# Turning input and output blocks in 32x32 squares on VectorE and DMA instead of with TensorE transposes

## The chip, the cores and the metric

The kernel runs on one core of a Trainium2 chip. The metric is the time of one execution on the device in microseconds; the median of three runs is compared.

## What is computed

`x` is 2 x 4096 x 192 (float32), 8192 rows of 192 features. Three stages follow each other:

```python
# attention: 8 heads of 24 features, 7 causal taps each
w = softmax(weight_gen, axis=-1)                  # (2, 4096, 8, 7)
out = einsum('bshk,bskhg->bshg', w, windows(x))   # sum of 7 shifted, weighted rows
# layer 1: 192 -> 1536 -> 192
h = (silu(out @ w_gate) * (out @ w_val)) @ w_out
# layer 2: 192 -> 2048 -> 192
z = h @ w_in
return (z * clip(z + 3, 0, 6) / 6) @ w_out2
```

## The kernel before

**Tiling.** Partition `p` holds the 64 consecutive rows `64p` to `64p + 63`. A block is `STEPS = 4` of these per partition, 512 rows; there are `BLOCKS = 16`. The taps' sum is made on VectorE with rows on the partitions (128 x 768, 4 rows of 192 features each). The matmuls want features on the partitions and the 512 rows as columns: a main tile of features 0 to 127 and a tail tile of features 128 to 191, which is kept in both halves of the partitions. So each block's input is turned once, and its output once in the other direction, since the result comes with features on the partitions (PSUM pair `acc[2]`) and is stored by rows.

**Numbers.** Each matmul operand is split in a rounded part (`hi`, made on ScalarE by a cast) and the rest (`lo`, made on VectorE by a subtraction), and three products are added. Matmuls use half of the array's rows (64 x 128), LOW and HIGH, two at a time. A hidden tile is 128 features of the 1536 (`N1 = 12` gated tiles, two up matmul sets and a product each) or of the 2048 (`N2 = 16` plain tiles).

**Periods.** Period `i` (1 to 15) runs the 12 gated tiles of block `i` and then the 16 plain tiles of block `i - 1`, in 8 steps of two tiles (`period`, L1295). Period 0 has gated tiles alone, period 16 plain tiles alone (`last_period`, L1322). Periods 2 to 14 are a loop on the engines (L293), the others are written out. The down matmuls run `LAG = 4` tiles behind the up matmuls, woven into the same steps (`gated_step` L1002, `plain_step` L1124); a step may begin when the hidden tiles of the step before the last are made (`up_ready`, L906).

**Order on the engines.** All orders are written out by hand. For tile `n` ScalarE makes silu or relu out of PSUM (`bend`, L448; it waits for the rest of tile `n - 2`, since `hidden` has two buffers), then the cast of tile `n - 1` (`round_hi`, L459). VectorE makes the product of tile `n` (`tile_product`, L715), then slot 0, then the rest of tile `n - 1` (`tile_lo`, L727), then slot 1 (`between`, L774). The slots hold the other work:

- the 18 operations of the next block's taps (`conv_op`, L664; the last two write `conv_main` and `conv_tail`, L709 and L711), in order from tile 0 on;
- in (6, 0) the fold of the output's tail (`fold_output`, L765), which moves the others back by one;
- in (10, 0) and (10, 1) the rest of layer 2's input (`input2_lo`, L754);
- in (11, 1), (12, 0) and (12, 1) the rest of layer 1's next input out of PSUM (`input1_lo`, L739): one operation of 512 columns and four of 256 on half the partitions;
- in (17, 1) the sum of layer 1's tail (`sum_tail`, L760).

ScalarE adds after tile 4 the copies of the output (`take_sum2`, L494, with `out_main`), after tile 9 the copies of the turned output out of PSUM (`take_rows`, L502), after tile 11 the casts of the next input (`input1_hi`, `input1_tail_hi`, L469 to L486), after tile 16 the copies of layer 1's sum (`take_sum1`, L488).

**TensorE's turning.** `transpose_output(i - 2)` (L1214) follows gated tile `ROWS_AFTER = 7`, `transpose_input(i + 1)` (L1179) follows the last gated tile; each is 8 transposes of the main part and 4 of the tail, half an array each, into PSUM. Block 0 is different: its seven products are added up and turned at once by matmuls with the identity (`turn_products0`, L1237). The last block's output is turned by `transpose_last` (L1197).

**SyncE.** In the loop it waits for the rows of block `i - 2`, stores them in one DMA (`store`, L358), waits for the taps of block `i + 1` and for the store, and loads the window of block `i + 2` (L380 to L385). GpSimd only makes the weights' rests in periods 0 and 1.

Of the kernel before, what the change touches and what calls it, by code (L numbers as in the profile page):

```python
# [35 lines left out]
P = 128  # L36
# [3 lines left out]
LAG = 4  # L40
FOLD_AT = 6
ROWS_AFTER = 7
# [4 lines left out]
def swiglu_hardswish_kernel(nc, x, taps_in, w_gate, w_val, w1_out, w2_in, w2_out, out):  # L47
# [69 lines left out]
    with ExitStack() as ctx:  # L117
# [26 lines left out]
        conv_main = sb("conv_main", [P, STEPS, P])  # L144
        conv_tail = sb("conv_tail", [P, STEPS, TAIL])
# [22 lines left out]
        ident = sb("ident", [P, P])  # L168
        last_tail = mid_tail
# [14 lines left out]
        s_window = sem("s_window")  # L184
        s_stage = [sem(f"s_stage{s}") for s in range(BUFFERS)]
# [15 lines left out]
        s_out_main = sem("s_out_main")  # L201
        s_out_rows = sem("s_out_rows")
        s_last_tail = sem("s_last_tail")
# [11 lines left out]
        s_conv_rows = sem("s_conv_rows")  # L215
# [4 lines left out]
        s_out_fold = sem("s_out_fold")  # L220
        s_mid = sem("s_mid")

        s_in_cols = sem("s_in_cols")
# [5 lines left out]
        s_out_t = sem("s_out_t")  # L229
# [12 lines left out]
        def by_half(ap):  # L242
            return ap.rearrange("p (t h q) -> p t h q", h=2, q=TAIL)

        def by_parity_half(ap):
            return ap.rearrange("p (a b h q) -> p a b h q", b=2, h=2, q=TAIL)

        def main_cols(banks):
            return banks[:, :, 0:STEPS * TAIL].rearrange("p h (t q) -> p t h q", q=TAIL)

        def tail_cols(banks, rows):
            return banks[rows, :, STEPS * TAIL:D * 2].rearrange("p h (a q) -> p a h q", q=TAIL)
# [3 lines left out]
        def input_banks(b):  # L256


            return acc_pair[1 if isinstance(b, int) and b == 0 else 2]

        def tails0():

            return acc_pair[2][halves[0], :, 0:STEPS * TAIL].rearrange("p h (t q) -> p t h q", q=TAIL)

        def output_banks(b):

            return acc_pair[1 if isinstance(b, int) and b >= BLOCKS - 2 else 2]
# [42 lines left out]
        def _(sp):  # L310
# [63 lines left out]
            sp.wait_ge(s_conv_rows, 1)  # L374
# [3 lines left out]
            sp.wait_ge(s_conv_rows, 2)  # L378
# [7 lines left out]
            for b in range(BLOCKS - 4, BLOCKS - 1):  # L386
                sp.wait_ge(s_out_rows, b + 1)
                store(b)
            sp.wait_ge(s_out_rows, BLOCKS)
            sp.wait_ge(s_last_rows, 2)  # L390
            store(BLOCKS - 1)
            sp.wait_ge(s_stored, 16 * BLOCKS)
# [34 lines left out]
        def _(act):  # L427
# [46 lines left out]
            def input1_tail_hi0():  # L474
                for half in halves:
                    last = nc.scalar.copy(by_half(inp[1]["tail_hi"][half, :]), tails0())
                last.then_inc(s_in1_hi, 1)

            def input1_tail_hi(b, par):
# [889 lines left out]
```

## Time and profile before

| | |
|---|---|
| median of 3 runs | 1233.72 us (1233.35 to 1233.98) |
| the profiled execution | 1232.71 us, its span 1230.9 us |
| TensorE busy | 1212.3 us (98%) |
| VectorE busy | 870.6 us (71%) |
| ScalarE busy | 662.6 us (54%) |
| GpSimd busy | 41.1 us (3%) |
| DMA packets | 12051, 32.01 MB |
| chain that ended last | TensorE 91%, VectorE 6%, ScalarE 2%, issue 1% |
| granted TensorE clock | 1.00 |

The profile follows one execution. Busy times are sums over the whole span; a matmul's own duration (0.39 us) is longer than the distance to the next, as they are pipelined and run two at a time. In a timeline the first number is the start in us, the second the time the instruction or merged group took, a number in brackets the idle time of its engine just before it and what ended that. The chain is followed back from the last instruction.

### The profile page before, as it was taken

To read this page: it belongs to the slowest core of one execution; us is meant where nothing else is said; L and a number is where in the kernel's file an instruction comes from. 1 tells how busy PE (TensorE), PEld (TensorE's weight loads), DVE (VectorE), ACT (ScalarE), POOL (GpSimd) and SP (SyncE) were. 2 spreads that over 40 slices of the span, in tenths; PEclk is the share of its full clock that TensorE was granted. 3 is DMA by queue.
4 is the path that set the end of the run, shared out by engine and by line. 5 is a ranking of instruction groups with operands and counts; after the bars stand their busy time and mean duration, and the time that the engine had idled before them with its cause. 6 is when DMAs were issued, how large, how long until landed. Compare 5 with 4: busy or idle time off the path is not lost.

```text
span 1230.9 us, 26836 instructions
## 1 busy us (share of the span) xinstructions
PE 1212.3 (98%) x10868; PEld 1025.1 (83%) x10868; DVE 870.6 (71%) x1349; ACT 662.6 (54%) x1185; POOL 41.1 (3%) x38
## 2 busy tenths in 40 slices
PE   8989999999999999999999999999999999999998
PEld 7767688889888888888889888898888888898976
DVE  4978786776868668686776868668686776864555
ACT  4455646556454554646556454554646556454555
POOL 4431000000000000000000000000000000000000
PEclk9999999999999999999999999999999999999999
DMA  6231001010100101001010100101001010000000
GB/s 179 97 101 33 1 8 39 2 46 1 46 2 1 46 1 46 1 9 39 1 46 1 46 1 1 46 1 46 1 8 38 1 46 1 14 1 2 14 12 16
DMA packets 12051, 32.01 MB, mean 26 GB/s; under 512 B 1078, under 2 KB 5942, under 8 KB 11828
## 3 DMA queue, kind: packets, MB, share of 16 engines
q1 hardware_dynamic: 11812, 30.42, 7.5%
q8 instruction: 86, 1.41, 0.5%
q10 hardware_dynamic: 144, 0.11, 0.0%
q14 instruction: 9, 0.07, 0.0%
HBM read 24.24 MB, written 6.29 MB: 25 GB/s over the span
## 4 chain that ended last, share of the span: by engine, by line
PE 91%; DVE 6%; ACT 2%; issue 1%; POOL 0%; ACTq 0%; POOLq 0%
PE up_bank L868 34%; PE acc L883 22%; PE up_bank L874 16%; PE acc L890 15%; DVE hid_lo L729 2%; PE up_bank L1234 1%; DVE hidden L724 1%; DVE prod_even L612 1%; DVE sum_even L616 1%; DVE hidden L721 1%; ACT hidden L456 1%; PE acc L1245 0%; PE acc L1251 0%; DVE sum_odd L616 0%; DVE prod_odd L612 0%
## 5 line engine op out<-in xcount | busy, mean ns | idle before, releaser
L868 PE MATMUL up_bank<-in_hi,up_hi 64*128 64x512 f32 x1280 | 355.3, 400 | 11.1 <-DVE hidden L721 6.4
L868 PE MATMUL up_bank<-in_lo,up_hi 64*128 64x512 f32 x1280 | 346.8, 387 | 0.0
L868 PE MATMUL up_bank<-in_hi,up_lo 64*128 64x512 f32 x1280 | 346.8, 387 | 0.0
L883 PE MATMUL acc<-hid_hi,dn_hi 64*128 64x512 f32 x872 | 337.5, 387 | 0.1
L890 PE MATMUL acc<-hid_hi,dn_tail 64*128 64x512 f32 x872 | 337.5, 387 | 0.1
L883 PE MATMUL acc<-hid_lo,dn_hi 64*128 64x512 f32 x872 | 337.1, 387 | 0.0
L890 PE MATMUL acc<-hid_lo,dn_tail 64*128 64x512 f32 x872 | 336.8, 386 | 0.0
L883 PE MATMUL acc<-hid_hi,dn_lo 64*128 64x512 f32 x872 | 336.8, 386 | 0.0
L724 DVE SCALAR_TENSOR_TENSOR hidden<-hidden,up_bank 128x512 f32<-128x512 f32 x256 | 175.8, 687 | 195.9 <-ACT hidden L456 195.5
L729 DVE TENSOR_TENSOR hid_lo<-hidden,hid_hi 128x512 fp32r<-128x512 f32 x448 | 312.7, 698 | 1.5 <-ACT hid_hi L463 0.5
L456 ACT ACTIVATE hidden<-up_bank,half_col 128x512 f32<-128x512 f32 x256 | 176.1, 688 | 227.9 <-DVE hid_lo L729 214.1
L454 ACT ACTIVATE hidden<-up_bank 128x512 f32<-128x512 f32 x192 | 115.0, 599 | 298.9 <-PE up_bank L874 245.4
L463 ACT CAST hid_hi<-hidden 128x512 fp32r<-128x512 f32 x448 | 273.7, 611 | 1.5 <-DVE hidden L724 0.8
L868 PEld LDWEIGHTS up_bank<-in_hi,up_hi 64*128 64x128 f32 x1280 | 195.8, 184 | 48.7 <-DVE hidden L721 18.4
L721 DVE TENSOR_TENSOR hidden<-hidden,up_bank 128x512 f32<-128x512 f32 x192 | 131.9, 687 | 123.2 <-ACT hidden L454 113.6
L868 PEld LDWEIGHTS up_bank<-in_lo,up_hi 64*128 64x128 f32 x1280 | 196.4, 184 | 21.8 <-DVE in_lo L743 0.4
L868 PEld LDWEIGHTS up_bank<-in_hi,up_lo 64*128 64x128 f32 x1280 | 196.7, 184 | 18.0
L874 PE MATMUL up_bank<-in_tail_hi,up_tail_hi 64*128 64x512 f32 x640 | 198.0, 387 | 0.0
L874 PE MATMUL up_bank<-in_tail_hi,up_tail_lo 64*128 64x512 f32 x640 | 197.9, 386 | 0.0
L874 PE MATMUL up_bank<-in_tail_lo,up_tail_hi 64*128 64x512 f32 x640 | 197.8, 386 | 0.0
L890 PEld LDWEIGHTS acc<-hid_hi,dn_tail 64*128 64x128 f32 x872 | 160.4, 184 | 14.5 <-PE acc L883 1.0
L883 PEld LDWEIGHTS acc<-hid_hi,dn_hi 64*128 64x128 f32 x872 | 160.5, 184 | 13.9 <-DVE hid_lo L729 0.5
(130 smaller groups left out, 1459.0 us busy)
## 6 DMA issues: line engine op xcount, KB each, us to landing
window<-in_x_dram SPq DMA_DIRECT2D x14, 960.0 KB
out_dram<-out_rows SPq DMA_DIRECT2D x16, 384.0 KB, 2.4
stage<-in_moe_w_out_dram SPq DMA_DIRECT2D x7, 384.0 KB, 3.5
taps<-in_weight_gen_dram SPq DMA_DIRECT2D x1, 1456.0 KB, 8.1
stage<-in_moe_w_in_dram SPq DMA_DIRECT2D x4, 256.0 KB, 4.2
window<-in_x_dram SPq DMA_DIRECT2D x2, 472.5 KB
window<-in_x_dram SPq DMA_DIRECT2D x2, 283.5 KB
stage<-in_moe_w_gate_dram SPq DMA_DIRECT2D x2, 256.0 KB, 6.4
```

The costliest lines, as they stand in the source:

```text
L454: nc.scalar.activation(buf, up_bank[2 * (n % 2)][:, :], ACT.Silu).then_inc(s_bent, 1)
L456: nc.scalar.activation(buf, up_bank[n % 4][:, :], ACT.Relu, bias=half_col[:, 0:1], scale=1.0 / 6.0).then_inc(s_bent, 1)
L463: nc.scalar.copy(hid_hi[:, n % RING, :], hidden[:, n % 2, :]).then_inc(s_hid_hi, 1)
L612: return nc.vector.tensor_tensor(by_head(dst[:, :]), by_head(window[:, j * D:(j + STEPS) * D]), w[:, :, j:j + 1].to_broadcast([P, HEADS, G ...
L616: return nc.vector.tensor_tensor(dst[:, :], dst[:, :], src[:, :], ALU.add)
L721: nc.vector.tensor_tensor(buf, buf, up_bank[2 * (n % 2) + 1][:, :], ALU.mult).then_inc(s_hidden, 1)
L724: nc.vector.scalar_tensor_tensor(out=buf, in0=buf, scalar=1.0, in1=up_bank[n % 4][:, :], op0=ALU.min, op1=ALU.mult).then_inc(s_hidden, 1)
L729: nc.vector.tensor_tensor(hid_lo[:, n % RING, :], hidden[:, n % 2, :], as_f32(hid_hi[:, n % RING, :]), ALU.subtract).then_inc(s_hid_lo, 1)
L868: return nc.tensor.matmul(dst[:, :], w[lane[half], col:col + P], a[lane[half], :], start=first and product == 0, stop=False)
L874: return nc.tensor.matmul(dst[:, :], w[lane[half], col:col + P], a[lane[half], :], start=False, stop=product == 2)
L883: return nc.tensor.matmul(acc[y][0], w[lane[half], k, :], a[lane[half], n % RING, :], start=half == LOW and product == 0 and k == 0, stop= ...
L890: return nc.tensor.matmul(acc[y][1], dn_tail[y][lane[half], k, :], a[lane[half], n % RING, :], start=half == HIGH and product == 0 and k == 0,
```

## The change

From block 2 on the input and, up to block 14, the output are turned without TensorE. VectorE's transpose turns every 32x32 square of a tile in place; the squares are then brought to their places by DMA.

- **Input.** Operation 17 of the taps writes the whole sum into `sum_even` in one add. VectorE turns it into `in_turned` (768 columns) in slot (11, 0). SyncE writes it to a scratch in DRAM with 4 DMAs (32 partitions, 6 runs of 512 bytes each), waits for them, and reads it back with 3 (`in_main`, which shares its memory with `out_main`, and `in_tail` in both halves). ScalarE casts the two whole tiles after tiles 21 and 22, VectorE makes the rests in slots (22, 1) and (23, 1).
- **Output.** VectorE turns `acc[2][0]` out of PSUM (512 columns) in slot (6, 1), and the folded tail (256 columns) in slot (7, 0). SyncE stores the squares with 24 DMAs a block, each 32 partitions with 4 runs of 128 bytes. The copies into `out_main` and out of the turned PSUM banks go.
- **Order.** The slots (6, 0), (6, 1), (7, 0) are kept for the output in every period, the taps' operations take the others. The two exponentials of the remaining taps in period 1 move from tiles 22 and 24 to 23 and 25. The window is loaded when the last product of the taps has read the old one. SyncE's loop is written out.
- **Blocks 0, 1 and 15.** TensorE turns on in blocks 0 and 1 (block 1 now with 8 + 8 transposes) and for the last output. Columns stand in another order (by square, then step), so some copies there have other access patterns.

```diff
-ROWS_AFTER = 7
+SQ = 32
...
-        conv_main = sb("conv_main", [P, STEPS, P])
-        conv_tail = sb("conv_tail", [P, STEPS, TAIL])
+        in_turned = sb("in_turned", [P, STEPS * D])
...
+        in_tail = sb("in_tail", [P, COLS])
+        in_main = out_main
+        turned_dram = nc.dram_tensor("turned_dram", (D, COLS), F32, kind="Internal").ap()
...
+        CONV_OPS = 17
+        LAST_PRODUCT = 15
+        BROUGHT = 3 * 16
+        STORES = (P // SQ) * (D // SQ) * 16
...
+            def bring_input(b):
+
+                by_feature = turned_dram.rearrange("(e f) (j c) -> f e j c", f=SQ, c=P)
+                for j in range(P // SQ):
+                    sp.dma_start(by_feature[:, :, j, :],
+                                 in_turned[j * SQ:(j + 1) * SQ, :].rearrange("f (e c) -> f e c", c=P)
+                                 ).then_inc(s_in_dram, 16)
+                sp.wait_ge(s_in_dram, (b - 1) * (P // SQ) * 16)
+                sp.dma_start(in_main[:, :], turned_dram[0:P, :]).then_inc(s_in_cols, 16)
+                for half in halves:
+                    sp.dma_start(in_tail[half, :], turned_dram[P:D, :]).then_inc(s_in_cols, 16)
+
             def store(b):
-                sp.dma_start(out_by_p[:, bass.ds(b * (STEPS * D), STEPS * D)], out_rows[:, :]).then_inc(s_stored, 16)
+
+                rows = out_by_p[:, bass.ds(b * (STEPS * D), STEPS * D)].rearrange("(j q) (t d) -> j q t d", q=SQ, t=STEPS)
+                for j in range(P // SQ):
+                    for e in range(D // SQ):
+                        if e < P // SQ:
+                            p0, at = e * SQ, j * P
+                        else:
+                            p0, at = j % 2 * TAIL + e * SQ - P, COLS + j // 2 * P
+                        sp.dma_start(rows[j, :, :, e * SQ:(e + 1) * SQ],
+                                     out_rows[p0:p0 + SQ, at:at + P].rearrange("q (t d) -> q t d", t=STEPS)
+                                     ).then_inc(s_stored, 16)
...
-            with sp.Fori(2, BLOCKS - 2) as i:
-                sp.wait_ge(s_out_rows, i - 1)
+            sp.wait_ge(s_in_turned, 1)
+            bring_input(2)
+            for i in range(2, BLOCKS - 2):
+                sp.wait_ge(s_out_turned, 2 * i - 2)
                 store(i - 2)
-                sp.wait_ge(s_conv_rows, i + 1)
-                sp.wait_ge(s_stored, 16 * i - 16)
+                sp.wait_ge(s_conv, i * CONV_OPS + LAST_PRODUCT)
+                sp.wait_ge(s_stored, i * STORES - STORES)
                 load_window(i + 2)
+                sp.wait_ge(s_in_turned, i)
+                sp.wait_ge(s_in1_lo, 2 * i + 2)
+                bring_input(i + 1)
...
             def input1_hi(b):
-                banks = input_banks(b)
-                act.wait_ge(s_in_cols, b + 1)
-                nc.scalar.copy(by_half(inp[1]["hi"][:, :]), main_cols(banks)).then_inc(s_in1_hi, 1)
...
+                act.wait_ge(s_in_cols, (b - 1) * BROUGHT)
+                act.wait_ge(s_val, b * N1)
+                nc.scalar.copy(inp[1]["hi"][:, :], in_main[:, :]).then_inc(s_in1_hi, 1)
+
+            def input1_tail_hi(b):
+                nc.scalar.copy(inp[1]["tail_hi"][:, :], in_tail[:, :]).then_inc(s_in1_hi, 1)
...
-                nc.scalar.copy(out_main[:, :], acc[2][0][:, :]).then_inc(s_out_main, 1)
-
-            def take_rows(b):
...
-                    if n == N1 - 1 and has_next and not fixed(i, 0):
+                    if n == N1 + 9 and has_next and not fixed(i, 0):
                         input1_hi(i + 1)
-                        input1_tail_hi(i + 1, 0)
-                        input1_tail_hi(i + 1, 1)
+                    if n == N1 + 10 and has_next and not fixed(i, 0):
+                        input1_tail_hi(i + 1)
...
+            def turn_input(b):
+
+                dve.wait_ge(s_conv, b * CONV_OPS)
+                nc.vector.transpose(in_turned[:, :].rearrange("p (e t q) -> p e t q", t=STEPS, q=SQ),
+                                    sum_even[:, :].rearrange("p (t e q) -> p e t q", t=STEPS, q=SQ)
+                                    ).then_inc(s_in_turned, 1)
...
+            def turn_output_main(b):
+
+                if isinstance(b, int):
+                    wait(dve, s_stored, b * STORES)
+                nc.vector.transpose(out_rows[:, 0:COLS], acc[2][0][:, :]).then_inc(s_out_turned, 1)
+
+            def turn_output_tail(b):
+                dve.wait_ge(s_out_fold, b + 1)
+                nc.vector.transpose(out_rows[:, COLS:], out_tail[:, :]).then_inc(s_out_turned, 1)
+
+            out_gaps = [(FOLD_AT, 0), (FOLD_AT, 1), (FOLD_AT + 1, 0)]
+            in2_gaps = [(N1 - 2, 0), (N1 - 2, 1)]
+            conv_gaps = [(n, slot) for n in range(N1) for slot in range(2) if (n, slot) not in out_gaps + in2_gaps]
...
-                if y == 2 and k == 0 and i < BLOCKS - 1:
-                    pe.wait_ge(s_in1_lo, 2 * i + 4)
-                elif y == 2 and k == 0 and i == BLOCKS - 1:
-                    pe.wait_ge(s_out_rows, i - 1)
+                if y == 2 and k == 0 and i == 1:
+                    pe.wait_ge(s_in1_lo, 4)
+                elif y == 2 and k == 0:
+                    pe.wait_ge(s_out_turned, 2 * i - 2)
...
-                    if n == ROWS_AFTER and i >= 2:
-                        transpose_output(i - 2)
-                if i + 1 < BLOCKS:
-                    transpose_input(i + 1)
```

## Rows read from the trace of the kernel before

**Rows 1.** Busy time by stretch: PE, PEld, DVE, ACT, POOL; clock, DMA share, GB/s.
```profile
555.00:592.00 37.00, 37.00 (x337) 33.30 (x335) 24.15 (x40) 21.77 (x39) 0.00 (x0) 1.00 0.08 27
```

**Rows 2.** Timeline of TensorE in gated steps, with output and with input turning.
```profile
540.73 0.39 PE L868 MATMUL up_bank<-in_hi,up_hi 64*128 64x512 f32 x2
...
543.90 0.40 PE L1220 MATMUL acc<-ident,out_main 64*128 64x64 f32 x8
...
547.54 0.39 PE L868 MATMUL up_bank<-in_hi,up_hi 64*128 64x512 f32 x2
...
483.17 0.40 PE L1186 MATMUL acc<-ident,conv_main 64*128 64x64 f32 x8
...
483.82 0.39 PE L868 MATMUL up_bank<-in_hi,up_lo 64*128 64x512 f32 x2
```

**Rows 3.** Timeline of TensorE where period 7 turns into period 8.
```profile
595.16 0.50 PE L868 MATMUL up_bank<-in_hi,up_hi 64*128 64x512 f32 x2
595.49 0.39 PE L868 MATMUL up_bank<-in_hi,up_lo 64*128 64x512 f32 x2
...
598.24 0.39 PE L883 MATMUL acc<-hid_lo,dn_hi 64*128 64x512 f32 x1
...
598.56 0.50 PE L868 MATMUL up_bank<-in_hi,up_hi 64*128 64x512 f32 x2
598.90 0.39 PE L868 MATMUL up_bank<-in_hi,up_lo 64*128 64x512 f32 x2
```

**Rows 4.** Timeline of ScalarE: relu of tiles 12 and 18 in periods 7 and 15.
```profile
560.20 0.69 ACT L456 ACTIVATE hidden<-up_bank,half_col 128x512 f32<-128x512 f32 x1 [0.41 <-PE up_bank L874]
...
574.59 0.69 ACT L456 ACTIVATE hidden<-up_bank,half_col 128x512 f32<-128x512 f32 x1 [0.93 <-DVE hid_lo L729]
...
1150.43 0.69 ACT L456 ACTIVATE hidden<-up_bank,half_col 128x512 f32<-128x512 f32 x1 [1.85 <-PE up_bank L874]
...
1163.99 0.69 ACT L456 ACTIVATE hidden<-up_bank,half_col 128x512 f32<-128x512 f32 x1 [0.85 <-DVE hid_lo L729]
```

**Rows 5.** Timeline of VectorE in gated tiles of period 8.
```profile
606.16 0.95 DVE L612 TENSOR_TENSOR prod_even<-window,taps 128x768 f32<-128x768 f32 x1
607.03 0.68 DVE L729 TENSOR_TENSOR hid_lo<-hidden,hid_hi 128x512 fp32r<-128x512 f32 x1
607.63 0.95 DVE L612 TENSOR_TENSOR prod_odd<-window,taps 128x768 f32<-128x768 f32 x1
608.69 0.69 DVE L721 TENSOR_TENSOR hidden<-hidden,up_bank 128x512 f32<-128x512 f32 x1
```

**Rows 6.** Timeline of VectorE and of TensorE in period 1, while GpSimd works.
```profile
90.78 1.90 DVE L612 TENSOR_TENSOR prod_even<-window,taps 128x768 f32<-128x768 f32 x1
...
90.91 0.51 PE L868 MATMUL up_bank<-in_hi,up_hi 64*128 64x512 f32 x2 [1.10 <-DVE hidden L721]
```

**Rows 7.** Timeline of SyncE's issues at the start, and the page's row of stores.
```profile
3.53 0.59 SPq L326 DMA_DIRECT2D stage<-in_moe_w_gate_dram  x1
4.16 0.58 SPq L364 DMA_DIRECT2D taps<-in_weight_gen_dram  x1
...
out_dram<-out_rows SPq DMA_DIRECT2D x16, 384.0 KB, 2.4
```

**Rows 8.** Timeline of VectorE (product of tile 7), ScalarE (relu of tiles 20, 21), period 8.
```profile
618.21 0.69 DVE L721 TENSOR_TENSOR hidden<-hidden,up_bank 128x512 f32<-128x512 f32 x1
...
652.67 0.69 ACT L456 ACTIVATE hidden<-up_bank,half_col 128x512 f32<-128x512 f32 x1 [0.93 <-DVE hid_lo L729]
...
654.79 0.69 ACT L456 ACTIVATE hidden<-up_bank,half_col 128x512 f32<-128x512 f32 x1 [0.93 <-DVE hid_lo L729]
```

**Rows 9.** Busy time by stretch around one weight load, one store, one window load.
```profile
84.30:92.00 7.70, 6.60 (x56) 4.78 (x56) 7.70 (x8) 3.55 (x7) 3.88 (x3) 1.00 0.18 51
...
626.00:629.30 3.30, 3.30 (x33) 2.71 (x30) 1.75 (x4) 1.26 (x3) 0.00 (x0) 1.00 0.30 119
628.80:633.00 4.20, 4.20 (x48) 3.45 (x48) 3.16 (x6) 2.34 (x6) 0.00 (x0) 1.00 0.69 234
```

More of the change, by code:

```diff
@@ L239, in of_pairs, with by_lane, squares_by_p, squares_by_t @@
             return ap.rearrange("p (a c) -> p a c", c=P)
[L242 to L252, printed above, removed]
-        halves = (slice(0, TAIL), slice(TAIL, P))
[L256 to L267, printed above, removed]
+        def by_lane(ap):
+            return ap.rearrange("p (h c) -> p h c", h=2)
+        def squares_by_p(ap):
+            return ap.rearrange("p (b t q) -> p b t q", t=STEPS, q=SQ)
+        def squares_by_t(ap):
+            return ap.rearrange("p (t b q) -> p b t q", t=STEPS, q=SQ)
+        halves = (slice(0, TAIL), slice(TAIL, P))
+        def main_banks(b):
+            return acc_pair[1 if b == 0 else 2][:, :, 0:STEPS * TAIL]
+        tail_banks = acc_pair[2][halves[0], :, STEPS * TAIL:]
+        def columns_of(banks, half, t):
+            return banks[:, half, :].rearrange("p (b t q) -> p b t q", t=STEPS, q=SQ)[:, :, t, :]
         def fixed(i, value):
@@ L531, in period @@
                         round_hi(i, n - 1)
[L532 to L533 removed]
+                    if fixed(i, 1) and n in (N1 + 11, N1 + 13):
+                        exponentials_rest((n - N1 - 11) // 2)
                     if isinstance(i, int) and (i, n) in splits_at:
@@ L616, in add @@
                 return nc.vector.tensor_tensor(dst[:, :], dst[:, :], src[:, :], ALU.add)
-            def to_rows(dst, first, last):
-                a, b = (v[:, :].rearrange("p (t d) -> p t d", t=STEPS)[:, :, first:last] for v in (sum_even, prod_even))
-                return nc.vector.tensor_tensor(dst[:, :, :], a, b, ALU.add)
             def normalise(w, k, done, base):
@@ L707, in conv_op @@
                     dve.wait_ge(s_conv, base + 16)
-                    last = to_rows(conv_main, 0, P)
-                else:
-                    to_rows(conv_tail, P, D).then_inc(s_conv_rows, 1)
-                    return
+                    last = add(sum_even, prod_even)
                 last.then_inc(s_conv, 1)
+            def turn_input(b):
[3 more added lines that the diff above has]
+                                    ).then_inc(s_in_turned, 1)
             def tile_product(i, n):
@@ L779, in between @@
                     k = n if n < LAG else LAG + 2 * (n - LAG) + slot
-                    if (n >= LAG or slot == 0) and k <= CONV_OPS:
+                    if (n >= LAG or slot == 0) and k < CONV_OPS:
                         if k == 0:
@@ L1235, in keep_warm, with add_turned @@
                                          start=True, stop=True)
+            def add_turned(k, rows, dims, banks):
+                for t in range(STEPS):
+                    for half in (LOW, HIGH):
+                        mm = nc.tensor.matmul(columns_of(banks, half, t), rows[lane[half], t, dims],
+                                              ident[lane[half], lane[half]], start=k == 0 and t == 0,
+                                              stop=k == K - 1 and t == STEPS - 1)
+                return mm
             def turn_products0():
@@ L1242, in turn_products0 @@
                     rows = first_products[k % len(first_products)][:, :].rearrange("p (t d) -> p t d", t=STEPS)
[L1243 to L1254 removed]
+                    add_turned(k, rows, slice(0, P), main_banks(0))
+                    mm = add_turned(k, rows, slice(P, D), tail_banks)
                     if k < K - 1:
```

201 lines of the change are left out of this document (76 added, 125 removed).

## The prediction

> **What bounds it now.** I read the busy table by stretch first: in a period of the steady loop TensorE is busy for 37.00 of 37.00 us at full granted clock, with VectorE at 24.15 and ScalarE at 21.77 [rows 1]. The reader is to see that only work of TensorE, or a gap in it, sets the time from period 2 to period 15; the other engines matter where they make it late. So the question is what the turning costs on TensorE's own stream, whether what takes its place stays beside the matmuls, and whether TensorE is waiting somewhere just below what a table of busy time shows.
>
> **Turning removed from TensorE.** The output turning of a block is one group of 8 + 4 transposes, the input turning another. A gated step without a group goes from 540.73 to 543.90, 3.17 us; the one with it from 543.90 to 547.54, 3.64 us [rows 2]. A group costs 0.47 us. For input, 483.17 to 483.82 covers the group and one pair of matmuls, 0.65 us; a pair follows the next in 3.17/14 = 0.226 us (28 half-array matmuls in the step, two at a time), so the group costs 0.43 us [rows 2]. Input groups of blocks 2 to 15 go (14), all on a full TensorE; output groups 0 to 13 likewise (14). The 15th output group, in the last period, stands ahead of a wait for ScalarE and VectorE anyway; I count nothing. Sum: 14 x 0.47 + 14 x 0.43 = 12.6 us. Block 1 gets 16 transposes for 12, some 0.1 us, against VectorE writing its sum in one add instead of two; nothing net.
>
> **The turn of the period.** The plain tiles are a ring between ScalarE and VectorE (relu, product, cast, rest, next relu) that runs at 654.79 - 652.67 = 2.12 us a tile [rows 8] against TensorE's 4.30/2 = 2.15 (19 pairs a plain step), so lateness once got is kept until the gated tiles. At the turn it reaches TensorE: 595.16 to 595.49 is 0.33, 598.24 to 598.56 is 0.32 and 598.56 to 598.90 is 0.34 where 0.226 is normal [rows 3]. That is 0.32 us a period, which the table calls busy. Now the lateness is partly made by the input work that the change moves: from relu of tile 12 to that of tile 18 it takes 574.59 - 560.20 = 14.39 us in a period that casts its next input at tiles 11 to 13, and 1163.99 - 1150.43 = 13.56 us in period 15, which has none [rows 4]. Of the 0.83 some 0.08 is the slower loop; 0.75 us is the casts. In the new kernel they are whole-tile copies at tiles 21 and 22 on ScalarE and whole-tile subtractions on VectorE in slot 1. There ScalarE is idle for 0.93 us before each relu [rows 4] and a copy takes about 0.5 us to the next start; VectorE has about 0.8 us and a 512-column operation takes 0.60 [rows 5]. So they cost nothing, and if the cover were gone each would cost its 0.5 or 0.6 us in the ring. A ring that is 0.75 us earlier clears a gap of 0.3. I take 0.3 x 13 turns = 3.9 us.
>
> **Added on VectorE.** Three turns a block: 512 and 256 columns in slots (6,1) and (7,0), 768 in (11,0). The trace has no such operation. Nearest rows: element operations of the same size, 0.87 us to the next start for 768 columns and 0.60 for 512 [rows 5]; from above, the same 768 columns when GpSimd shares the port, 1.90 us [rows 6]; a price below the plain add would gain nothing, as that time is spare. I take the plain rows, the same number of elements read and written. Two 768-column operations per tile fit now: the product follows 0.19 us after its predecessor is through (1.06 from 607.63 to 608.69 against 0.87) [rows 5]. Tile 6 then holds fold and 512 columns where it held fold and 768; tile 7 holds 256 and 768 for 768 and 768; tile 11 holds 768 alone. No step is fuller than before. At 1.90 for 768 (1.27 for 512) tile 6 ends 0.2 us late and relu of tile 12 about 0.3 late: at worst the 3.9 us are lost again. ScalarE loses three copies to out_main and out_rows; it was not the bound.
>
> **Added on SyncE and the DMA queues.** A store becomes 24 DMAs of 128 packets of 128 bytes: 3072 packets, 192 for each of 16 queues. Issues follow each other at 4.16 - 3.53 = 0.63 us [rows 7], so 24 take 15.1 us. In the frame of period 8: the tail turn follows the product at 618.21 [rows 8], done at 619.2; issue until 634.3; landing 2.4 more [rows 7], 636.7; then SyncE lets the window go, whose 960 KB take 4.2 us at 234 GB/s [rows 9], to 641.5; the four input DMAs (issued by 640.4) land about 644; three read-backs are issued in 1.9 and land 648.3. ScalarE wants them after relu and cast of tile 21, 654.79 + 1.1 = 655.9 [rows 8]. Slack 7.6 us. SyncE serves nothing else here; the next window is wanted only in the next period.
> A 128-byte packet is not in the trace. From below, a 768-byte packet: share 0.18 of 16 queues over 7.70 us for 512 packets, 43 ns [rows 9], 8.3 us for 192, hidden behind the issue. From above, the 3072-byte packets of the present store: 0.30 x 3.30 x 16 / 128 = 124 ns [rows 9], 23.8 us, so 8.7 later than the issue and 1.1 past the slack, about what the ring's regained 0.75 us absorbs. I take the lower, since a sixth of those bytes is nearer to 768 than to 3072: cost nothing.
>
> **Period 1.** It stalls on VectorE, behind two 768-column operations per tile beside GpSimd: 1.10 us idle at 90.91, and once more the same at tile 8 [rows 6]. The new slots leave tiles 6 and 7 three empty slots there, so VectorE catches up and the second goes; the first stays. I take 1.2 us, with a little for the input casts that leave the start of its plain tiles.
>
> **Sum.** 12.6 + 3.9 + 1.2 = 17.7 us off the profiled execution's 1232.71 (span 1230.9): 1215.0. The median of the runs stands 1.01 above that execution: 1216.0. The last period is as before: fold and the two turns there, 1.9 us, lie beside TensorE's first two plain up steps, 18 pairs or 4.1 us.
>
> **Rivals.**
> (a) *Only the transposes.* The gap at the turn is not lateness but the price of a wait as such, and stays; period 1 gives little. For it: the bubbles are as small as a refill. Against: period 15 is early by 0.75. Time 1233.7 - 12.6 - 0.6 = 1220.5.
> (b) *The squares are late.* Place: ScalarE's wait for the read-back at tile 21, in front of every relu behind it, so TensorE stops. Price: 192 packets beyond (15.1 + 7.6 + 1)/192 = 0.123 us each; the change's 1.2 us a period is used up at 0.13 us. At 0.15 us (28.8 us) it is 5 us late a period, 14 periods, 70 us: 1233.7 - 17.7 + 70 = 1286, slower. For it: the only packet into the output that is measured takes 124 ns, and that stands at the edge. Against: most of those 124 ns are bytes, as 43 ns for a quarter of the size says.
> The Trainium skill (DMA: Bandwidth & Descriptors, Specifications) speaks against the change here: a transfer under 512 bytes makes the DMA engine read, modify and write. No row shows one. If that doubled a 43 ns packet it would be 86 ns and still hidden.
> (c) *VectorE is the bound.* A turn at a quarter of an add's speed (2.5 us for 512, 3.5 for 768) makes tile 6 1.4 late, adds 1.5 at tile 11, and TensorE waits some 1 to 3 us a period: 1229 to 1255. Against: nothing in the rows costs so much but beside GpSimd, and GpSimd does nothing in the loop [rows 1].
> That it does not do what it says is out of question for blocks 2 to 14; in 0, 1 and 15 TensorE goes on turning, which is in the sum.
>
> **Numbers.** Forecast 0.62, (a) 0.18, (b) 0.12, (c) 0.06 (half of it still faster), 0.02 for a new wait that I do not see. The range holds forecast and (a) with the unknown of period 1: 1212.5 (both gaps of period 1, the last output group and 1 us of what else its stalls hold) to 1222.5; the rest lies above it. A difference under 0.2% (2.5 us) cannot be told from none. Faster 0.84 (forecast, (a), 0.03 of (c), 0.01 of (b)), same 0.03, slower 0.13.
>
> **What would show it.** Period from 73.8 to about 72.6 us; gated and plain steps at 3.17 and 4.30; no 0.33 spacings at the turn of the period; VectorE's turn of 768 columns near 0.95 us; from last store issue to landing 2 to 3 us; ScalarE's wait for in_main absent from the table of waits. Wrong it is if ScalarE waits for DMA at tile 21, if issues of squares are much farther apart than 0.63 us, or if TensorE waits for VectorE at tiles 6 to 12.

## The result and the profile after

The changed kernel takes **1212.99 us** (median of 4 runs, 1212.69 to 1213.09), the kernel before beside it 1233.53 us (1233.16 to 1233.98): ratio 0.9833, 95% interval 0.9816 to 0.985, 20.5 us less. The profiled execution took 1212.99 us, its span is 1211.2. The page of the changed kernel:

```profile
PE 1194.2 (99%) x10524; PEld 1067.7 (88%) x10524; DVE 880.5 (73%) x1334; ACT 631.2 (52%) x1096; POOL 41.7 (3%) x38
...
DMA packets 77636, 44.87 MB, mean 37 GB/s; under 512 B 54246, under 2 KB 69862, under 8 KB 77412
...
q1 hardware_dynamic: 77396, 43.29, 13.4%
...
HBM read 31.58 MB, written 11.80 MB: 36 GB/s over the span
```

TensorE has lost 18.1 us of busy time and still fills 99% of the span, so it is the bound as before. VectorE has gained 9.9 us and the queue has over six times the packets (11812 before); TensorE stays as full as it was.

**The period.** In periods 2 to 14 ScalarE loads a table once, at the first tile, and that row dates the period. The timeline of ScalarE, in the kernel before and then in the changed one:

```profile
521.92 1.28 ACT L454 ACT_TABLE_LOAD   x1 [0.91 <-DVE hid_lo L729]
...
595.80 1.28 ACT L454 ACT_TABLE_LOAD   x1 [0.91 <-DVE hid_lo L729]
```
```profile
512.01 1.28 ACT L492 ACT_TABLE_LOAD   x1 [0.91 <-DVE hid_lo L739]
...
584.66 1.28 ACT L492 ACT_TABLE_LOAD   x1 [0.91 <-DVE hid_lo L739]
```

73.88 us became 72.65. Over the twelve periods from 2 to 13 it is (1038.92 - 152.65)/12 = 73.856 before and (1020.35 - 149.18)/12 = 72.598 after: 1.258 us each, 15.1 us in all. Up to the first of these loads 3.5 us went (152.65 against 149.18), behind the last of them 1.1. The first periods differ a little from the rest, so runs are compared below by the even period, the mean over the last nine of the twelve (5 to 13): 73.854 before and 72.616 after, 1.24 us less.

**The turn of the period** [rows 3]. The waits of TensorE's weight loads between 160 and 1060 us, before and then after (columns: us in total, times, longest):

```profile
PEld up_bank L868 <- DVE hidden L721: 4.2, 12, 0.4
PEld up_bank L868 <- DVE hidden L724: 3.0, 12, 0.3
```
```profile
PEld up_bank L891 <- issue: 2.2, 13, 0.2
```

Two waits for VectorE's product stood at each turn and are gone; what is left is no wait for another engine ("issue"). On TensorE's timeline the pairs there follow each other at 0.23 us, where [rows 3] had 0.33:

```profile
584.66 0.42 PE L891 MATMUL up_bank<-in_hi,up_hi 64*128 64x512 f32 x2
584.89 0.42 PE L891 MATMUL up_bank<-in_hi,up_lo 64*128 64x512 f32 x2
```

**The turns on VectorE** beside the plain rows of [rows 5]; timeline of the changed kernel, tiles 6, 7 and 11:

```profile
533.78 0.72 DVE L782 STREAM_TRANSPOSE out_rows<-acc 128x512 f32<-128x512 f32 x1
534.75 0.69 DVE L731 TENSOR_TENSOR hidden<-hidden,up_bank 128x512 f32<-128x512 f32 x1 [0.25 <-ACT hidden L492]
535.36 0.44 DVE L786 STREAM_TRANSPOSE out_rows<-out_tail 128x256 f32<-128x256 f32 x1
...
548.05 0.97 DVE L721 STREAM_TRANSPOSE in_turned<-sum_even 128x768 f32<-128x768 f32 x1
548.94 0.65 DVE L739 TENSOR_TENSOR hid_lo<-hidden,hid_hi 128x512 fp32r<-128x512 f32 x1
```

A turn of 768 columns is 0.97 us beside 0.95 for the sum or product of that size, and 0.89 to the next start, beside 0.87.

**The squares.** SyncE's timeline, and when ScalarE takes the input (with [rows 7, 8]):

```profile
535.82 12.61 SPq L382 DMA_DIRECT2D out_dram<-out_rows  x24
...
556.37 0.34 SPq L369 DMA_DIRECT2D out_main<-turned_dram  x1
556.75 2.41 SPq L371 DMA_DIRECT2D in_tail<-turned_dram  x2
```
```profile
570.83 0.62 ACT L517 CAST in_hi<-out_main 128x512 fp32r<-128x512 f32 x1
```

24 issues take 12.61 us, 0.525 each; a store's issue has landed after 1.5 us (median, the page's section of issues). Busy by stretch (columns as in [rows 1]) shows the queues during them and where the read-back ends:

```profile
536.00:548.50 12.50, 12.50 (x113) 12.12 (x112) 10.84 (x16) 4.42 (x8) 0.00 (x0) 1.00 0.19 31
...
561.00:575.00 14.00, 14.00 (x128) 13.21 (x126) 9.16 (x15) 9.38 (x17) 0.00 (x0) 1.00 0.00 1
```

The 16 queues are busy for 0.19 of the time with the squares, so a packet of 128 bytes costs 0.19 x 12.5 x 16 / 3072 = **12.4 ns** of a queue. From 561 on they are still; the cast that wants the data starts at 570.83 and its row shows no wait. The slack is 10 us.

**The start.** Timeline of TensorE up to period 2, first before, then after (the wait at 90.91 is in [rows 6]):

```profile
62.74 0.46 PE L1186 MATMUL acc<-ident,conv_main 64*128 64x64 f32 x8 [0.99 <-DVE conv_tail L621]
...
102.86 0.50 PE L868 MATMUL up_bank<-in_hi,up_hi 64*128 64x512 f32 x2 [1.10 <-DVE hidden L721]
```
```profile
61.96 0.46 PE L1207 MATMUL acc<-ident,sum_even 64*128 64x64 f32 x8 [0.30 <-DVE sum_even L628]
...
90.08 0.50 PE L891 MATMUL up_bank<-in_hi,up_hi 64*128 64x512 f32 x2 [1.11 <-DVE hidden L731]
```

The wait at 102.86 is gone, that of the opening is 0.7 us shorter.

### The profile page after: what moved, and what is told of

It reads as the page before. It is cut to its first block, busy times and chain, and to the rows that moved or that the text cites. A ratio compares the mean times of both kernels' runs of the same rounds, so it can differ in the third digit from the quotient of the medians.

```text
span 1211.2 us, 26409 instructions
## 1 busy us (share of the span) xinstructions
PE 1194.2 (99%) x10524; PEld 1067.7 (88%) x10524; DVE 880.5 (73%) x1334; ACT 631.2 (52%) x1096; POOL 41.7 (3%) x38
## 3 DMA queue, kind: packets, MB, share of 16 engines
HBM read 31.58 MB, written 11.80 MB: 36 GB/s over the span
## 4 chain that ended last, share of the span: by engine, by line
PE 92%; DVE 5%; ACT 2%; issue 1%; DMA 0%; ACTq 0%
PE up_bank L891 34%; PE acc L906 23%; PE up_bank L897 17%; PE acc L913 16%; DVE hid_lo L739 1%; PE acc L1242 1%; DVE hidden L734 1%; DVE prod_even L624 1%; DVE hidden L731 1%; DVE sum_even L628 0%; ACT hidden L494 0%; DMA taps<-in_weight_gen_dram 0%; DVE prod_odd L624 0%; DVE taps L301 0%; DVE tap_max L610 0%
## 5 line engine op out<-in xcount | busy, mean ns | idle before, releaser
L891 PE MATMUL up_bank<-in_lo,up_hi 64*128 64x512 f32 x1280 | 353.1, 387 | 0.0
L891 PE MATMUL up_bank<-in_hi,up_lo 64*128 64x512 f32 x1280 | 353.0, 387 | 0.0
L734 DVE SCALAR_TENSOR_TENSOR hidden<-hidden,up_bank 128x512 f32<-128x512 f32 x256 | 176.1, 688 | 199.7 <-ACT hidden L494 199.7
L891 PEld LDWEIGHTS up_bank<-in_hi,up_hi 64*128 64x128 f32 x1280 | 198.9, 184 | 37.5 <-DVE hidden L731 12.2
L891 PEld LDWEIGHTS up_bank<-in_lo,up_hi 64*128 64x128 f32 x1280 | 199.1, 184 | 14.3 <-DVE in_lo L744 0.4
L891 PEld LDWEIGHTS up_bank<-in_hi,up_lo 64*128 64x128 f32 x1280 | 199.2, 184 | 12.5
L897 PE MATMUL up_bank<-in_tail_hi,up_tail_hi 64*128 64x512 f32 x640 | 202.6, 386 | 0.0
L897 PE MATMUL up_bank<-in_tail_hi,up_tail_lo 64*128 64x512 f32 x640 | 202.5, 386 | 0.0
L897 PE MATMUL up_bank<-in_tail_lo,up_tail_hi 64*128 64x512 f32 x640 | 202.5, 386 | 0.0
```

Source lines behind the costliest of these rows:

```text
L734: nc.vector.scalar_tensor_tensor(out=buf, in0=buf, scalar=1.0, in1=up_bank[n % 4][:, :], op0=ALU.min, op1=ALU.mult).then_inc(s_hidden, 1)
L891: return nc.tensor.matmul(dst[:, :], w[lane[half], col:col + P], a[lane[half], :], start=first and product == 0, stop=False)
L897: return nc.tensor.matmul(dst[:, :], w[lane[half], col:col + P], a[lane[half], :], start=False, stop=product == 2)
```

## The experiments

Theory: the transposes give two thirds of the gain; the gap at the turn of the period is lateness of the ring between ScalarE and VectorE and gives the rest of each period; the squares are hidden by their slack. Rivals: it is all transposes; the gap is a price of the turn itself; VectorE or the queues are at their edge. Each run stands against the kernel whose edit it is: the changed kernel at 1212.99, or the kernel before, measured beside the run (1233.53 for both of its edits).

**What a group of transposes costs.** `g1`, `g2`: in the changed kernel, behind the last gated tile of periods 2 to 14:
```diff
+            def extra_groups(i, count):
+                pe.wait_ge(s_out_turned, 2 * i - 2)
+                for _ in range(count):
+                    for m in range(2 * STEPS + STEPS):
+                        half = m % 2
+                        nc.tensor.transpose(acc_pair[2][:, half, m // 2 * TAIL:(m // 2 + 1) * TAIL],
+                                            ident[lane[half], :], ident[lane[half], lane[half]])
...
+                if not fixed(i, 1) and not fixed(i, BLOCKS - 1):
+                    extra_groups(i, 1)           # g2: 2
```


> The changed kernel, with one group of twelve transposes of the identity (as many and as large as the turning of one block) put back on TensorE at the end of the gated steps of periods 2 to 14; nobody reads them. What it tells: what one group costs on a TensorE that is full, with nothing for ScalarE, VectorE or DMA attached to it. Theory (a group costs its own 0.43 to 0.47 us): 13 x 0.43 to 0.47 = 5.6 to 6.1 us more than the changed kernel, 1218.6 to 1219.1. Rival (a group disappears in small gaps of TensorE): under 1.5 us more.

> The same with two groups, as many transposes as the change takes from a period. Theory: 26 x 0.43 to 0.47 = 11.2 to 12.2 us more than the changed kernel, 1224.2 to 1225.2, with no gap at the turn of the period, so that it stands still some 7 to 9 us below the kernel before: that rest is not the transposes'. Rival (what the change gave is all the transposes', which cost more than I took): about 1232. Other rival (lateness of the ring comes back with them): a gap of 0.3 us each period, 1228 to 1229.

Measured 1217.82 and 1222.91: +4.83 and +9.92, 0.37 and 0.38 us a group. By the table loads the even period is 72.994 and 73.377, so 0.38 a group in both. Both lie below the expected ranges (5.6 to 6.1 and 11.2 to 12.2), but the kind is the theory's, two groups cost twice one; 1232 and 1228 are both out. So as many transposes as the change took out of periods 2 to 14 give back half of the 20.5 us only.

**The same removed from before.** `b_noturn`: the kernel before without transposes in periods 2 to 14; input and output of those blocks aren't turned. The work of ScalarE, VectorE and the queues stays; ScalarE's waits for the transposes (L469, L502) now stand for what came before these.
```diff
-                    if n == ROWS_AFTER and i >= 2:
+                    if n == ROWS_AFTER and i == BLOCKS - 1:
                         transpose_output(i - 2)
...
-                if i + 1 < BLOCKS:
+                if i == 1:
                     transpose_input(i + 1)
```


> The kernel before with the transposes of TensorE left out in periods 2 to 14 (26 groups) and everything of ScalarE, VectorE and the queues kept, so input and output of those blocks are not turned. Theory: 26 x 0.43 to 0.47 = 11.2 to 12.2 us less than the kernel before, 1221.3 to 1222.3, and the gap of 0.3 us at the turn of each period, where TensorE waits for VectorE's result, stays (12 or 13 waits at the lines of the gated product). Rival (transposes and gap are one thing): the gap goes too and the time is 1217 to 1218. A mixed case: with 0.9 us less of TensorE in a period ScalarE and VectorE, which are no faster, have less room, and the gap grows: then above 1222.3.

Measured 1222.50 (1221.57 to 1223.13), 11.03 less than before: 0.424 us for each of 26 groups, just below the range that I gave. The weight loads' waits (160 to 1060 us):

```profile
PEld up_bank L874 <- DVE hidden L727: 4.2, 12, 0.4
PEld up_bank L874 <- DVE hidden L730: 3.2, 12, 0.3
```

Both waits stand where they stood. The even period is 73.003: of the 1.24 us the transposes are 0.85, and 0.39 is something else.

**Whether the casts make the gap.** `b_fewcasts`: the kernel before with the input's casts and rests of periods 2 to 14 cut to 8 columns (the next input isn't renewed there).
```diff
-                        input1_hi(i + 1)
-                        input1_tail_hi(i + 1, 0)
-                        input1_tail_hi(i + 1, 1)
+                        if isinstance(i, int):
...
+                        else:
+                            act.wait_ge(s_in_cols, i + 2)
+                            nc.scalar.copy(inp[1]["hi"][:, 0:8], acc_pair[2][:, 0, 0:8]).then_inc(s_in1_hi, 2)
```


> The kernel before with TensorE's transposes kept, but in periods 2 to 14 the copies of the next input by ScalarE and the subtractions by VectorE at tiles 11 to 13 are cut to one of 8 columns each, so the next block's input isn't renewed. Theory (the copies and subtractions make the ring between ScalarE and VectorE late, which shows as a gap at the turn of the period): 0.3 x 13 = 3.9 us less than the kernel before, 1229.6, and no wait of TensorE's for VectorE in the loop. Rival (the gap is the price of a wait or of the turn itself): the same time within 0.5 us, the gap stays.

Measured 1227.84, 5.69 less. No wait of the weight loads is left between 160 and 1060 us, the even period is 73.452 us, 0.40 less. TensorE does the same work in both; the gap was lateness, and it was larger than I took. How much larger shows between the same two matmuls on TensorE's timeline, around the turn from period 7 to 8, in the kernel before and then in `b_fewcasts`:

```profile
593.10 0.39 PE L868 MATMUL up_bank<-in_hi,up_hi 64*128 64x512 f32 x1
...
599.83 0.39 PE L868 MATMUL up_bank<-in_hi,up_hi 64*128 64x512 f32 x1
```
```profile
590.87 0.39 PE L876 MATMUL up_bank<-in_hi,up_hi 64*128 64x512 f32 x1
...
597.22 0.39 PE L876 MATMUL up_bank<-in_hi,up_hi 64*128 64x512 f32 x1
```

6.73 us against 6.35. The three spacings of [rows 3] hold 0.31 of these 0.38 us; the rest lies in hundredths between the other matmuls.

`a_casts`: the other way, the changed kernel with that work at tiles 11 to 13 again, beside what it does at tiles 21 to 23:
```diff
+                    if n == N1 - 1 and not isinstance(i, int):
...
+                        nc.scalar.copy(inp[1]["hi"][:, :], mid_main[:, :])
+                        for at in (0, COLS // 2):
+                            for half in halves:
+                                last = nc.scalar.copy(inp[1]["tail_hi"][half, at:at + COLS // 2], out_tail[half, :])
```
The matching subtractions stand on VectorE in slots (11, 1), (12, 0), (12, 1).


> The changed kernel with the work of tiles 11 to 13 put back beside what it has: on ScalarE one 512-column copy and four 256-column copies of half the lanes after tile 11, on VectorE one 512-column subtraction and four of 256 columns at tiles 11, 12 and 12, in the loop's periods; their results are written over by the real input at tiles 21 and 22. Theory (this work at these tiles is what made the ring late at the turn of the period): TensorE waits 0.3 us for VectorE at each turn again, 13 x 0.3 = 3.9 us more than the changed kernel, 1216.9. Rival (the gap went for another reason): within 0.7 us of the changed kernel. A reason for more: the changed kernel's period is 1.2 us shorter, so ScalarE and VectorE have less room: up to 1 us a period, 1226.

Measured 1219.20, +6.2. Waits of the weight loads, and on the timeline the two of one turn:

```profile
PEld up_bank L908 <- DVE hidden L740: 4.0, 12, 0.4
PEld up_bank L908 <- DVE hidden L743: 3.4, 12, 0.3
...
513.74 0.19 PEld L908 LDWEIGHTS up_bank<-in_hi,up_hi 64*128 64x128 f32 x2 [0.29 <-DVE hidden L743]
...
517.15 0.19 PEld L908 LDWEIGHTS up_bank<-in_hi,up_hi 64*128 64x128 f32 x2 [0.32 <-DVE hidden L740]
```

The gap is back, 0.52 us in the even period (73.133), and +6.2 lies between my 3.9 and my 13. It comes in two parts, 3.4 us apart: the late product, and once more at the next step, as in the kernel before (595.16 and 598.56 in [rows 3]). It is larger than the 0.39 there, perhaps because here the work is added, where there it stood in place of the later casts; that was not tried.

**How near VectorE stands to its edge.** `turn2`: the output turn of 512 columns and the input turn done twice; `turnout2`: the output turn alone.
```diff
-                nc.vector.transpose(out_rows[:, 0:COLS], acc[2][0][:, :]).then_inc(s_out_turned, 1)
+                nc.vector.transpose(out_rows[:, 0:COLS], acc[2][0][:, :]).then_inc(s_first_out, 1)
+                dve.wait_ge(s_first_out, b + 1)
+                nc.vector.transpose(out_rows[:, 0:COLS], acc[2][0][:, :]).then_inc(s_out_turned, 1)
```


> The changed kernel with two of VectorE's three turns (output, 512 columns, and input, 768 columns) done twice: 1.7 us more of VectorE in each period. Theory (VectorE has that much room in tiles 6 to 12): within 0.5 us of the changed kernel. Rival (the turns stand at the edge, and what they cost is what the change lost): TensorE waits at tiles 6 to 12, 0.3 to 1.5 us a period, 4 to 20 us more.

> The changed kernel with only the output turn of 512 columns done twice (0.6 us more of VectorE at tile 6; the run with this and the input turn doubled was 6.9 us above the changed kernel). Theory (the input turn at tile 11 stands where the ring has nothing to give, the output turn at tile 6 has two tiles of 0.25 and 0.69 us idle behind it): within 0.5 us of the changed kernel, so the 6.9 us are the input turn's. Rival (any addition on VectorE from tile 6 on makes the ring late at the turn): 5 to 7 us more, with TensorE's two waits at the turn of the period.

`turn2` 1219.87, +6.9: my theory fell. The size is the rival's, but not the place: no wait stands at tiles 6 to 12, they stand at the turn of the period. `turnout2` 1212.96, +0.0: the theory of the second run holds. Waits of `turn2`, and its timeline of VectorE at tile 11:

```profile
PEld up_bank L899 <- DVE hidden L740: 4.3, 12, 0.4
PEld up_bank L899 <- DVE hidden L737: 4.0, 12, 0.4
...
550.72 0.97 DVE L723 STREAM_TRANSPOSE in_turned<-sum_even 128x768 f32<-128x768 f32 x1
551.73 0.98 DVE L727 STREAM_TRANSPOSE in_turned<-sum_even 128x768 f32<-128x768 f32 x1
```

With one input turn at tile 11 TensorE has no wait; a second, on top of the doubled output turn, brings the two waits of `a_casts` back, with the same 0.52 us a period (73.132). The edge thus lies less than 1.01 us (550.72 to 551.73) of VectorE's work at tile 11 behind the kernel as it is. The output turn alone does not do it: at tile 6, with 0.25 us idle behind it and 0.69 a tile later, 0.6 us more are absorbed. The input turn was not doubled alone.

**How near the squares stand to theirs.** `st48`, `st60`: 48 and 60 squares a block for 24, the added ones into scratch.
```diff
-                for j in range(P // SQ):
+                for m in range(P // SQ + AGAIN):      # AGAIN = 4, 6
+                    j = m % (P // SQ)
```


> The changed kernel with 48 square stores per block for 24, the second 24 into a scratch tensor. Issues stand 0.525 us apart, so the read-back of the input comes 12.6 us later; it had landed at 560.5 and was wanted at 573.0 in the same period. Theory (hidden by 12 us, issue sets the pace): at the edge, within 2 us of the changed kernel, and a wait for in_main begins to show. Rival (the queues or HBM are the limit and contend with the loads): clearly slower, 10 us or more. Other rival (nobody waits for these stores): no change at all, and none with 60.

> The same with 60 square stores per block: the read-back 18.9 us later, 6 to 7 us past the point where ScalarE wants it in each of some 12 periods. Theory: 60 to 90 us more than the changed kernel, 1275 to 1300, with ScalarE waiting for in_main before tile 22 of each period. Rival (there is more slack than I read from the trace, or the transfers are not in the way): under 10 us.

`st48` 1227.07 (1224.14 to 1231.75, +14.1), `st60` 1316.77 (1308.62 to 1321.69, +103.8). Both theories missed in size: they allowed 2 us and 60 to 90, and the first number lies where the rival (queues or HBM as the limit, 10 us or more) put it. ScalarE's waits for the read-back, `st48` and then `st60`:

```profile
ACT in_hi L522 <- DMA in_tail<-turned_dram: 22.3, 12, 3.8
```
```profile
ACT in_hi L522 <- DMA in_tail<-turned_dram: 104.3, 13, 9.7
```

Both expectations start from a slip of mine: 573.0 was read as the point where the input is wanted, but that is the cast of the tail; the first cast starts at 570.83. With a slack of 10 us instead of 12, 48 squares (12.6 later) should be late by 2 to 3 us and 60 (18.9 later) by 8 to 9. Measured: 1.9 and 8.0 us a wait in the mean. The issues keep their distance (24 and 24 take 12.50 and 12.41 us in `st48`), and the queues are busy for 0.21 of the second 24 (550.7 to 563 us). So the number of issues sets the pace, the place of the wait is the one named, and a queue at its limit does not show. `st48`'s waits vary from 0.25 to 3.77 us a period at that even pace, and its executions by 0.6%; what varies behind the issues was not tried. Of its 1.9 us a period TensorE sees 1.12 (73.72 against 72.60 over the twelve periods), with the turn's gap in it.

`st60` costs more than TensorE's own waits. The view of its waits, and busy by stretch around one of them:

```profile
PE acc L911 <- DVE hid_lo L744: 69.1, 14, 7.0
```
```profile
538.60:543.20 4.60, 0.05 (x2) 0.00 (x0) 1.33 (x3) 2.23 (x4) 0.00 (x0) 0.72 0.22 57
543.20:544.50 1.30, 1.28 (x5) 0.83 (x5) 1.07 (x2) 1.19 (x2) 0.00 (x0) 0.50 0.00 0
...
546.00:547.50 1.50, 1.50 (x10) 1.13 (x10) 1.29 (x2) 0.59 (x2) 0.00 (x0) 0.52 0.00 0
547.50:549.00 1.50, 1.50 (x16) 1.30 (x14) 0.76 (x2) 1.20 (x2) 0.00 (x0) 1.00 0.00 0
```

After 4.57 us of idleness (538.65 to 543.22) TensorE works at a granted clock of 0.50, 1.2 GHz, for 4.3 us. The pairs follow each other at 0.42 us there instead of 0.23, so about 2 us are lost behind such a wait. For a dozen waits that is some 24 us, an estimate; with the 69.1 and the turn's gap (12 x 0.52) it makes some 99 of the 108.7 us that the profiled execution, the slowest of the four, lies above the changed kernel.

**Period 1 and the opening.** `p1slots`: in period 1 the taps' operations start in before's slots, without the three empty ones:
```diff
+                if fixed(i, 1) and 2 * n + slot <= CONV_OPS:
+                    if 2 * n + slot < CONV_OPS:
+                        conv_op(2, 2 * n + slot)
+                    else:
+                        turn_input(2)
```
`split`: block 1's last addition as two, of 512 and 256 columns, in the same slot.
```diff
-                    last = add(sum_even, prod_even)
+                    if fixed(b, 1):
...
+                        nc.vector.tensor_tensor(a[:, :, 0:P], a[:, :, 0:P], c[:, :, 0:P], ALU.add)
+                        last = nc.vector.tensor_tensor(a[:, :, P:D], a[:, :, P:D], c[:, :, P:D], ALU.add)
```


> The changed kernel with period 1's sums and products of the taps back in the slots that the kernel before used (tiles 6 and 7 get no empty slot), the turn of the input behind them at tile 8. Theory (three empty slots let VectorE catch up beside GpSimd in period 1, and that is the second wait of 1.1 us which the kernel before shows at tile 8): TensorE waits there again, 1.1 us more than the changed kernel. Rival (the wait went for another reason, for instance since VectorE no longer works for the input at the start of the plain tiles): the same within 0.3 us.

> The changed kernel with the last addition of block 1's taps written as two, of 512 and of 256 columns, as the kernel before has it. Theory (what I had counted at nothing was this: in block 1's opening TensorE waits for VectorE's sum, 0.99 us before and 0.30 us after): 0.3 to 0.7 us more than the changed kernel. Rival: the same within 0.2 us, and the opening's wait is shorter for another reason.

`p1slots` 1214.77, +1.8 us where 1.1 was expected. TensorE's timeline has the second wait back:

```profile
90.22 0.50 PE L898 MATMUL up_bank<-in_hi,up_hi 64*128 64x512 f32 x2 [1.11 <-DVE hidden L731]
...
102.18 0.50 PE L898 MATMUL up_bank<-in_hi,up_hi 64*128 64x512 f32 x2 [1.10 <-DVE hidden L731]
```

`split` 1213.00, nothing: the theory is out. VectorE's timeline says why. First `split`, then the kernel before:

```profile
61.07 0.68 DVE L717 TENSOR_TENSOR sum_even<-sum_even,prod_even 128x512 f32<-128x512 f32 x1
61.67 0.41 DVE L718 TENSOR_TENSOR sum_even<-sum_even,prod_even 128x256 f32<-128x256 f32 x1
```
```profile
61.07 0.68 DVE L621 TENSOR_TENSOR conv_main<-sum_even,prod_even 128x512 f32<-128x512 f32 x1
61.67 0.68 DVE L729 TENSOR_TENSOR hid_lo<-hidden,hid_hi 128x512 fp32r<-128x512 f32 x1
62.27 0.41 DVE L621 TENSOR_TENSOR conv_tail<-sum_even,prod_even 128x256 f32<-128x256 f32 x1
```

Two additions in a row end nearly as soon as one of 768 (TensorE waits 0.36 us for 0.30). What the kernel before paid for was that a tile's rest stood between them, as each operation has a slot of its own: the last sum started at 62.27 instead of 61.67. By these rows the opening's 0.7 us are a slot saved, not an operation; no run put the slot back.

**A faster one.** `spread`: period 1's maxima and shifts of the taps one to a tile.
```diff
-                if fixed(i, 1) and N1 + 6 <= n < N1 + 6 + HALF:
+                if fixed(i, 1) and N1 + 1 <= n < N1 + 1 + PARTS and slot == 1:
...
+                    part = n - N1 - 1
...
-                elif fixed(i, 1) and N1 + 6 + HALF <= n < N1 + 6 + PARTS:
+                elif fixed(i, 1) and N1 + 6 <= n < N1 + 6 + PARTS and slot == 1:
+                    part = n - N1 - 6
```


> An attempt at a faster kernel: the changed kernel with period 1's four maxima of the taps in slot 1 of tiles 13 to 16 and its four shifts in slot 1 of tiles 18 to 21, where the changed kernel has all eight in both slots of tiles 18 to 21, which keeps VectorE full from 123 to 136 us. Expected: TensorE's waits between 125 and 149 us get shorter, 1 to 3 us less than the changed kernel, 1210 to 1212. Rival (the exponentials and their table loads on ScalarE set those waits): the same within 0.5 us.

Measured **1209.54 us**, 3.45 less than the changed kernel and below the range I gave: ratio to before 0.9802 (0.9788 to 0.9815). TensorE's waits between 84 and 149 us, after and then `spread`:

```profile
PE up_bank L891 <- DVE hidden L734: 1.6, 4, 0.5
PE up_bank L891 <- DVE hidden L731: 1.5, 2, 1.1
```
```profile
PE up_bank L891 <- DVE hidden L731: 1.5, 2, 1.1
PE up_bank L891 <- DVE hidden L734: 0.3, 1, 0.3
```

The waits in the plain tiles (L734) go from 1.6 to 0.3 us, and those of the gated tiles, beside GpSimd's work, stay. That is 1.3 of the 3.45 us. The rest doesn't show as idle time of TensorE, whose recorded matmuls overlap. It shows in what TensorE gets done: between 112 and 153 us it starts 356 matmuls in `spread` and 328 in the changed kernel (weight loads busy 37.46 and 32.07 us). At 28 matmuls in 3.17 us these 28 are 3.2 us. The rival is out: ScalarE's exponentials stayed at their tiles and the time fell.

## Why the prediction was right

It said 1216.0 (range 1212.5 to 1222.5, faster 0.84); it was 1212.99, 3 us below and near the lower end. The mechanism held, and the experiments show its two main terms one by one. In size the largest term was a little large and the others small, so part of the good sum is luck.

| term | predicted | measured | from |
|---|---|---|---|
| 28 groups of transposes | 12.6 | 28 x 0.424 = 11.9 | `b_noturn`; 28 x 0.38 = 10.6 by `g1`, `g2` |
| gap at 13 turns | 3.9 | 13 x 0.39 = 5.1 | even periods of `b_noturn` and after; `b_fewcasts` 5.7 |
| period 1's slots | 1.2 | 1.8 | `p1slots` |
| opening of block 1 | 0 | 0.7 | waits 0.99 and 0.30; `split` rules out the operation |
| turns on VectorE | 0 | 0 | `turnout2`; no wait of TensorE's at tiles 6 to 12 of the loop |
| squares | 0 | 0 | slack 10 us; no wait of ScalarE's for them |
| sum | 17.7 | 19.5 of 20.5 | 18.2 with `g1`, `g2` |

- **Transposes.** 0.47 and 0.43, read as distances between rows of one step, were 0.424 over 26 groups taken out and 0.38 for groups put in; the difference of these two was not looked into. Rival (a) is out: the transposes alone give 11.0 of 20.5 us in the loop.
- **The gap.** This is the term that was most mis-sized: 0.32 us was read by adding up the three clearly stretched spacings at both places of one turn. The step as a whole is 0.38 longer than in `b_fewcasts`, as shown there, and the even period 0.39 to 0.40. The weight loads' waits are no measure of the loss either: 4.2 + 3.0 us in 12 periods are 0.6 a period. Cause and condition (casts at tiles 11 to 13) are shown from both sides, by `b_fewcasts` and `a_casts`. That the loss is 0.52 us both for the casts put back and for a second input turn is seen, not explained.
- **VectorE.** The forecast took the plain add (0.95) for a turn, and the rows have 0.97. The Trainium skill (Vector Engine (DVE) Microarchitecture Reference, on the reshape front-end) says the 32x32 transpose is pipelined to one element per cycle and lane. By that a turn would take no longer than another pass over as many columns, by my estimate, and the trace agrees (0.971 us in the mean for 768 columns, beside 0.951 to 0.993 for the sums and products). Rival (c) is out. Its bound was of use: the forecast's "at worst the 3.9 us are lost again", for turns at 1.90 us, is what happened in `turn2`, at 6.9.
- **Squares.** Pitch 0.525 us where I took 0.63 from two issues at the start; 24 in 12.6 us, and a slack of 10 for 7.6. The packet was bounded by 43 and 124 ns and was 12.4, below the lower end: neither bound had been scaled down to 128 bytes (a sixth of the 43 ns is 7). Rival (b) needed (12.6 + 10)/192 = 0.118 us a packet and is nearly ten times away, but by the number of issues it is near: `st48` is what it looks like.
- The Trainium skill (DMA: Bandwidth & Descriptors, Specifications) has a transfer under 512 bytes read, modified and written. The bytes of the page can't decide that here: HBM reads grew by 31.58 - 24.24 = 7.34 MB and writes by 5.5, which is just what the 14 read-backs of 512 KB and the 14 scratch copies ask for. What the trace decides is the price that the prediction weighed with it: a packet of 128 bytes took 12.4 ns, not 43 or 86.
- **Period 1** was right in its place and small in size, 1.8 us for 1.2. Of what is left, 1 us or more, a part lies behind 126 us, where before waits 0.48 and 2.07 us (at 136.77 and 143.45) and after five times, 1.8 us in all. The input's casts and the exponentials both moved there; neither was tried by itself.

## What to carry over

When the bound engine is nearly always busy, look at the waits of its weight loads: a wait too short for the busy table was worth a quarter of this gain, and it was caused by work on other engines some 35 us earlier. Take its size from a whole period, not from the few spacings that catch the eye. Work moved off the bound engine costs nothing only at its place: a second output turn was free at tile 6, and with a second input turn at tile 11 the gap was back; double each added piece alone to learn that. With many small DMAs, count issues before bytes, and compare their sum with the slack to the first reader, not to the last.

## What the hardware showed

- A 128-byte packet from SBUF to HBM took 12.4 ns of a queue, 3072 of them ran inside the issue of 24 DMAs, 0.525 us apart.
- A 32x32 turn on VectorE takes little more than a sum: 971 ns for 768 columns beside 951 to 993, 717 for 512 out of PSUM beside 681 to 698.
- After 4.57 us without a matmul TensorE was granted 0.50 (1.2 GHz) for 4.3 us in `st60`, with pairs 0.42 us apart instead of 0.23. Around the wait of 1.10 us at 90.91 the granted clock is 1.00 [rows 6, 9].
- A group of 12 small transposes, two at a time, lengthens a full TensorE's period by 0.38 to 0.43 us.
